# Block 0's convolution as five sets of turned products instead of seven, with a new order of the first loads

## The reference

```python
w = exp(weight_gen - max); w = w / (sum(w) + 1e-09)      # over the 7 taps
out[b, s, h, :] = sum_k w[b, s, h, k] * x_pad[b, s + k, h, :]   # 6 rows of zeros in front
```

## Time and profile before

| what | us |
|---|---|
| median of 3 runs | 1212.82 |
| the profiled execution, its own time | 1212.99 |
| its span, first to last instruction | 1211.2 |
| TensorE (PE) busy in the span | 1194.2 |
| VectorE (DVE) busy | 880.5 |
| ScalarE (ACT) busy | 631.2 |
| GpSimd (POOL) busy | 41.7 |

### The profile page before, as it was taken

One profiled execution on the slowest core, in us unless ns is written; L12 is line 12 of the kernel. 1 busy time (PEld: TensorE's weight loads), 2 busy tenths in 40 slices (PEclk: granted clock), 3 DMA queues, 4 the chain that ended last, 5 costly groups with the idle time before them and its releaser, 6 DMA issues.

```text
span 1211.2 us, 26409 instructions
## 1 busy us (share of the span) xinstructions
PE 1194.2 (99%) x10524; PEld 1067.7 (88%) x10524; DVE 880.5 (73%) x1334; ACT 631.2 (52%) x1096; POOL 41.7 (3%) x38
## 2 busy tenths in 40 slices
PE   8999999999999999999999999999999999999998
PEld 7768789999988998999899988888989899998876
DVE  5887796776868778686776868778686776865565
ACT  4455645546364554645546364554645546364555
POOL 4431000000000000000000000000000000000000
PEclk9999999999999999999999999999999999999999
DMA  6332002020110202002020110202002020100000
GB/s 180 103 99 64 1 10 69 1 77 1 27 51 4 74 1 62 17 10 68 1 77 1 17 61 4 75 1 60 18 10 68 1 77 2 22 24 4 11 10 18
DMA packets 77636, 44.87 MB, mean 37 GB/s; under 512 B 54246, under 2 KB 69862, under 8 KB 77412
## 3 DMA queue, kind: packets, MB, share of 16 engines
q1 hardware_dynamic: 77396, 43.29, 13.4%
q10 hardware_dynamic: 144, 0.11, 0.0%
HBM read 31.58 MB, written 11.80 MB: 36 GB/s over the span
## 4 chain that ended last, share of the span: by engine, by line
PE 92%; DVE 5%; ACT 2%; issue 1%; DMA 0%; ACTq 0%
PE up_bank L891 34%; PE acc L906 23%; PE up_bank L897 17%; PE acc L913 16%; DVE hid_lo L739 1%; PE acc L1242 1%; DVE hidden L734 1%; DVE prod_even L624 1%; DVE hidden L731 1%; DVE sum_even L628 0%; ACT hidden L494 0%; DMA taps<-in_weight_gen_dram 0%; DVE prod_odd L624 0%; DVE taps L301 0%; DVE tap_max L610 0%
## 5 line engine op out<-in xcount | busy, mean ns | idle before, releaser
L891 PE MATMUL up_bank<-in_hi,up_hi 64*128 64x512 f32 x1280 | 356.6, 392 | 9.3 <-DVE hidden L731 5.3
L891 PE MATMUL up_bank<-in_lo,up_hi 64*128 64x512 f32 x1280 | 353.1, 387 | 0.0
L891 PE MATMUL up_bank<-in_hi,up_lo 64*128 64x512 f32 x1280 | 353.0, 387 | 0.0
L906 PE MATMUL acc<-hid_hi,dn_hi 64*128 64x512 f32 x872 | 337.3, 387 | 0.3 <-DVE hid_lo L739 0.2
L913 PE MATMUL acc<-hid_hi,dn_tail 64*128 64x512 f32 x872 | 337.3, 387 | 0.1
L906 PE MATMUL acc<-hid_lo,dn_hi 64*128 64x512 f32 x872 | 336.8, 386 | 0.0
L913 PE MATMUL acc<-hid_lo,dn_tail 64*128 64x512 f32 x872 | 336.8, 386 | 0.0
L906 PE MATMUL acc<-hid_hi,dn_lo 64*128 64x512 f32 x872 | 336.8, 386 | 0.0
L734 DVE SCALAR_TENSOR_TENSOR hidden<-hidden,up_bank 128x512 f32<-128x512 f32 x256 | 176.1, 688 | 199.7 <-ACT hidden L494 199.7
L739 DVE TENSOR_TENSOR hid_lo<-hidden,hid_hi 128x512 fp32r<-128x512 f32 x448 | 310.9, 694 | 1.0
L494 ACT ACTIVATE hidden<-up_bank,half_col 128x512 f32<-128x512 f32 x256 | 176.4, 689 | 226.4 <-DVE hid_lo L739 163.4
(11 more groups left out here) (117 smaller groups left out, 1398.8 us busy)
## 6 DMA issues: line engine op xcount, KB each, us to landing
window<-in_x_dram SPq DMA_DIRECT2D x14, 960.0 KB
out_dram<-out_rows SPq DMA_DIRECT2D x360, 16.0 KB, 1.5
turned_dram<-in_turned SPq DMA_DIRECT2D x56, 96.0 KB, 4.6
out_main<-turned_dram SPq DMA_DIRECT2D x14, 256.0 KB, 2.8
in_tail<-turned_dram SPq DMA_DIRECT2D x28, 128.0 KB, 3.0
stage<-in_moe_w_out_dram SPq DMA_DIRECT2D x7, 384.0 KB, 3.5
taps<-in_weight_gen_dram SPq DMA_DIRECT2D x1, 1456.0 KB, 8.5
stage<-in_moe_w_in_dram SPq DMA_DIRECT2D x4, 256.0 KB, 4.4
```

What stands on the lines that cost most here:

```text
L891: return nc.tensor.matmul(dst[:, :], w[lane[half], col:col + P], a[lane[half], :], start=first and product == 0, stop=False)
L906: return nc.tensor.matmul(acc[y][0], w[lane[half], k, :], a[lane[half], n % RING, :], start=half == LOW and product == 0 and k == 0, stop= ...
```

## The change

- The seven products reach TensorE as five sets: taps 6, 5 and 4 alone, then the sums of 3 and 2 and of 1 and 0. Of a pair the first product goes to PSUM (`z`, in the banks `up_bank2` and `up_bank3`, now one tile `up_pair1`), the second to SBUF, and VectorE adds them in SBUF. The normalised taps lie behind `z`, half of them in each of the two banks.
- Product order is now from the last tap to the first. The halo comes in two parts of 3 rows, near and far, each by one DMA a batch; tap 5 waits for the near part, the pair (3, 2) for the far one.
- The taps of block 0 are issued by SP ahead of the window instead of by ScalarE.
- No warm-up slot between the sets; `WARM_SLOTS` is 10 instead of 16.
- ScalarE casts weight pieces 0 to 4 before it reads the banks (before: 0 to 2, then the exponentials for blocks 1 and 2 and the Silu table, then 3 and 4), then piece 5, these exponentials, the table, and piece 6.
- `shift_early` follows the whole of block 0's convolution on VectorE.
- SP's load of block 1's window waits for the fifth set.

```diff
-WARM_SLOTS = 16
+WARM_SLOTS = 10
...
-        up_bank = [ctx.enter_context(nc.psum_tensor(f"up_bank{u}", [P, COLS], F32)) for u in range(4)]
+        up_pair = [ctx.enter_context(nc.psum_tensor(f"up_pair{u}", [P, 2, COLS], F32)) for u in range(2)]
+        up_bank = [up_pair[u // 2][:, u % 2, :] for u in range(4)]
...
-        first_taps = up_bank[3][:, 0:TAPS]
+        SUMS, TAPS2 = STEPS * D // 2, TAPS // 2
+
+        def sums_in(pair):
+            return pair[:, :, 0:SUMS].rearrange("p a (h g) -> p a h g", g=G)
+
+        def taps_in_banks(pair):
+            return pair[:, :, SUMS:SUMS + TAPS2].rearrange("p a (h k) -> p a h k", k=K)
+
+        def by_step_pair(ap):
+            return ap.rearrange("p (a h g) -> p a h g", a=2, g=G)
+
+        first_sets = [(6,), (5,), (4,), (3, 2), (1, 0)]
...
             def load_window0():
 
+                sp.dma_start(taps[:, 0:TAPS], taps_by_p[:, 0:TAPS]).then_inc(s_taps0, 16)
                 sp.dma_start(window[:, HALO * D:], x_by_p[:, 0:STEPS * D]).then_inc(s_window0, 16)
-                for e in range(B):
-                    p0, row0 = e * BATCH_P, e * S
-                    rows = x_rows[row0 + TPP - HALO:row0 + TPP - HALO + (BATCH_P - 1) * TPP, :]
-                    sp.dma_start(window[p0 + 1:p0 + BATCH_P, 0:HALO * D],
-                                 rows.rearrange("(p t) d -> p (t d)", t=TPP)[:, 0:HALO * D]).then_inc(s_halo0, 16)
+                for first, landed_halo in ((HALO // 2, s_halo_near), (0, s_halo_far)):
+                    for e in range(B):
+                        p0, row0 = e * BATCH_P, e * S + TPP - HALO + first
+                        rows = x_rows[row0:row0 + (BATCH_P - 1) * TPP, :].rearrange("(p t) d -> p (t d)", t=TPP)
+                        sp.dma_start(window[p0 + 1:p0 + BATCH_P, first * D:(first + HALO // 2) * D],
+                                     rows[:, 0:HALO // 2 * D]).then_inc(landed_halo, 16)
...
-            sp.wait_ge(s_product0, K)
+            sp.wait_ge(s_set0, len(first_sets))
...
-            act.dma_start(taps[:, 0:TAPS], taps_by_p[:, 0:TAPS]).then_inc(s_taps0, 16)
             act.wait_ge(s_half, 1)
             nc.scalar.activation(warm[:, 0:1], half_col[:, :], ACT.Exp)
             act.wait_ge(s_shifted, 1)
             exponentials(0, TAPS)
-            for q in range(3):
+            for q in range(OWN - 2):
                 weight_hi(q)
+            input1_hi_banks(0)
+            weight_hi(OWN - 2)
             act.wait_ge(s_shifted, 2)
             exponentials(TAPS, EARLY * TAPS)
             nc.scalar.activation(warm[:, 1:2], half_col[:, :], ACT.Silu)
-            for q in range(3, OWN - 2):
-                weight_hi(q)
-            input1_hi_banks(0)
-            for q in range(OWN - 2, OWN):
-                weight_hi(q)
+            weight_hi(OWN - 1)
             periods(act, period)
...
+                z, zt = sums_in(up_pair[1]), taps_in_banks(up_pair[1])
...
-                product(w_psum, K - 1, first_products[0]).then_inc(s_product0, 1)
-                dve.wait_ge(s_halo0, B * 16)
-                dve.wait_ge(s_halo_zero, 2)
-                for k in range(1, K):
-                    if k == K - 1:
-                        shift_early()
+
+                def product0(j, dst):
+                    return nc.vector.tensor_tensor(dst, by_step_pair(window[:, j * D:(j + STEPS) * D]),
+                                                   zt[:, :, :, j:j + 1].to_broadcast([P, 2, HEADS // 2, G]), ALU.mult)
+
+                for k, members in enumerate(first_sets):
+                    rows = by_step_pair(first_products[k % len(first_products)][:, :])
+                    if k == 0:
+                        dve.wait_ge(s_window0, 16)
+                    if members[0] == HALO - 1:
+                        dve.wait_ge(s_halo_near, B * 16)
+                        dve.wait_ge(s_halo_zero, 2)
+                    if members[-1] == HALO // 2 - 1:
+                        dve.wait_ge(s_halo_far, B * 16)
                     wait(dve, s_turned0, k - len(first_products) + 1)
-                    product(w_psum, k - 1, first_products[k % len(first_products)]).then_inc(s_product0, 1)
+                    if len(members) == 1:
+                        product0(members[0], rows).then_inc(s_set0, 1)
+                    else:
+                        dve.wait_ge(s_set0, k)
+                        product0(members[0], z).then_inc(s_part0, 1)
+                        product0(members[1], rows).then_inc(s_part0, 1)
+                        dve.wait_ge(s_part0, 2 * (k - 2))
+                        nc.vector.tensor_tensor(rows, z, rows, ALU.add).then_inc(s_set0, 1)
...
             conv_block0()
+            shift_early()
             input1_lo_banks(0)
...
-                for k in range(K):
-                    pe.wait_ge(s_product0, k + 1)
+                for k in range(len(first_sets)):
+                    pe.wait_ge(s_set0, k + 1)
                     rows = first_products[k % len(first_products)][:, :].rearrange("p (t d) -> p t d", t=STEPS)
                     add_turned(k, rows, slice(0, P), main_banks(0))
                     mm = add_turned(k, rows, slice(P, D), tail_banks)
-                    if k < K - 1:
+                    if k < len(first_sets) - 1:
                         mm.then_inc(s_turned0, 1)
-                        keep_warm(1)
```

More of the change, by code:

```diff
@@ L183, in swiglu_hardswish_kernel @@
         s_window0 = sem("s_window0")
-        s_halo0 = sem("s_halo0")
+        s_halo_near = sem("s_halo_near")
+        s_halo_far = sem("s_halo_far")
         s_taps_rest = sem("s_taps_rest")
@@ L215, in swiglu_hardswish_kernel @@
         s_norm0 = sem("s_norm0")
-        s_product0 = sem("s_product0")
+        s_part0 = sem("s_part0")
+        s_set0 = sem("s_set0")
         s_turned0 = sem("s_turned0")
@@ L656, in conv_block0 @@
                 dve.wait_ge(s_norm0, 3)
-                w_psum = first_taps.rearrange("p (c k) -> p c k", k=K)
-                nc.vector.tensor_tensor(w_psum, w, denom[:, :].unsqueeze(2).to_broadcast([P, HEADS, K]),
-                                        ALU.mult).then_inc(s_norm0, 1)
+                z, zt = sums_in(up_pair[1]), taps_in_banks(up_pair[1])
+                nc.vector.tensor_tensor(zt, w.rearrange("p (a h) k -> p a h k", a=2),
+                                        denom[:, :].rearrange("p (a h) -> p a h", a=2).unsqueeze(3).to_broadcast(
+                                            [P, 2, HEADS // 2, K]), ALU.mult).then_inc(s_norm0, 1)
@@ L660, in conv_block0 @@
                 dve.wait_ge(s_norm0, 4)
-                dve.wait_ge(s_window0, 16)
-                product(w_psum, K - 1, first_products[0]).then_inc(s_product0, 1)
-                dve.wait_ge(s_halo0, B * 16)
-                dve.wait_ge(s_halo_zero, 2)
-                for k in range(1, K):
-                    if k == K - 1:
-                        shift_early()
-                    wait(dve, s_turned0, k - len(first_products) + 1)
-                    product(w_psum, k - 1, first_products[k % len(first_products)]).then_inc(s_product0, 1)
+                def product0(j, dst):
+                    return nc.vector.tensor_tensor(dst, by_step_pair(window[:, j * D:(j + STEPS) * D]),
+                                                   zt[:, :, :, j:j + 1].to_broadcast([P, 2, HEADS // 2, G]), ALU.mult)
@@ L1243, in add_turned @@
                                               ident[lane[half], lane[half]], start=k == 0 and t == 0,
-                                              stop=k == K - 1 and t == STEPS - 1)
+                                              stop=k == len(first_sets) - 1 and t == STEPS - 1)
                 return mm
             def turn_products0():
-                for k in range(K):
-                    pe.wait_ge(s_product0, k + 1)
+                for k in range(len(first_sets)):
+                    pe.wait_ge(s_set0, k + 1)
                     rows = first_products[k % len(first_products)][:, :].rearrange("p (t d) -> p t d", t=STEPS)
```

## The result

| | before | changed |
|---|---|---|
| median, us | 1212.82 (8 runs) | 1207.44 (8 runs) |
| lowest to highest | 1212.50 to 1213.08 | 1207.12 to 1210.69 |
| profiled execution, its own time | 1212.99 | 1208.50 |
| its span | 1211.2 | 1206.4 |
| mean granted clock of that span | 1.000 | 0.998 |

The ratio is 0.9961, with a 95% interval of 0.9950 to 0.9972: 0.4% faster, as forecast in sign and nearly in size (1208.0). What was not forecast is the spread. Five runs lie between 1207.12 and 1207.58 at a clock of 0.999 or 1.000, and three at 1208.50, 1209.61 and 1210.69 with 0.998, 0.997 and 0.997.

A forecast was written before the change was run, and what follows sets the result against it. The prediction took TensorE to set the pace at the start, up to the banks' reading at 21.83 us. It summed 1212.99 - 5.15 + 0.36 = 1208.2, less 0.17: 1208.0 us, range 1206.7 to 1210.4.

The forecast's parts named there:

- Step 1: Start, block 0's taps: they land at 3.6 us instead of 5.06, so the first product starts at 6.35.
- Step 2: Halo in two parts: near half needs no wait at 7.2 us; far half is awaited until 9.3.
- Step 3: VectorE's products and adds: adds take 0.95 us each, bounded by 1.90; the pairs are ready at 12.1 and 14.9.
- Step 4: TensorE's sets: banks full at 16.65 us instead of 21.80, 5.15 gained, 1.3 idle before the fifth set.
- Step 5: ScalarE's list behind the banks: first Silu waits for ScalarE, 0.36 us late; GpSimd's later weights stay hidden.
- Step 6: After the start: the shift is kept through 62 us and beyond; one VectorE-GpSimd meeting more or less is 0.95 us.
- Rivals A and B: A: first DMAs no faster, 1209.1 us, chance 0.15; B: gain partly given back at 15 to 62 us, 1209.9, 0.13.
- Rival C: TensorE's clock stays low or falls in the gaps: 11 us lost against 4.8 gained, 1219 us, chance 0.04.

The follow-up runs named there:

- e9: e5 with 18 warm-up slots ahead of the first set and two after the fourth: 1209.24 us, ratio 0.9970.
- e6: Changed kernel with the halo in one part, waited for ahead of the second product: 1215.16 us, ratio 1.0016.
- e3: Changed kernel with ScalarE's casts of weights 5, 6 and 7 moved after the second Silu and the first rounding: 1210.22 us.
- e8: Changed kernel with the first product of each pair in an SBUF tile instead of PSUM: 1210.02 us, ratio 0.9977.
- e12: The changed kernel itself, measured again: 1208.51 us, ratio 0.9965.
- e2: Changed kernel with 16 warm-up slots instead of 10: 1208.12 us, ratio 0.9962.
- e7: Changed kernel with seven single sets without adds instead of five sets: 1209.62 us, ratio 0.9976.
- e11: Changed kernel with one warm-up slot after the first and fourth sets each, and ScalarE's casts of weights 5 to 7 moved again: 1208.86 us, ratio 0.9967.
- e1: Changed kernel with two warm-up slots after the fourth set: 1208.05 us, ratio 0.9964.
- e4: Changed kernel with the later casts of e3 and the filled gap of e1 together: 1209.56 us.
- e5: Changed kernel with block 0's taps issued by ScalarE's queue again: 1215.79 us, ratio 1.0018.
- e10: The kernel before the change with 10 warm-up slots instead of 16: 1224.18 us, ratio 1.0074.

## Why the prediction was right, and where its sizes were off

**Step 1** (taps at 3.6): right in kind, too late by 0.7 us. They land at 2.86 (0.73 + 2.13), at the lower bound of 2.8. The estimate by the Trainium skill's page "DMA: Bandwidth & Descriptors", 3.0, was the nearer one, though the page gives its table for DMAs that GpSimd issues. The text held that an earlier landing would change nothing, as the far halo would be awaited: that was the error, next step. e9 prices the landing at 1.4 to 2.0 us.

**Step 2** (near half in time, far half awaited at 9.3): the near half was in time, the far half too. Both products behind it started without a wait for a DMA at 6.48 and 8.40; taking 9.3 as the far half's landing, from the undivided halo's 9.11, was too cautious. In e6 the undivided halo itself is in by 8.00. Why it comes earlier is not shown: the taps have left the second queue, and the weights behind the halo are issued 1.2 us later (3.15 against 1.95). The margin is small, as the profile of e3 has a wait of 0.17 us for the far half.

**Step 3** (adds at 0.95): measured 0.96 in PSUM and 1.81 and 1.40 in SBUF (e8); the upper bound of 1.90 was the price of the form that the change avoids. Two starts were mis-sized, as each pair waits for the end of the set before it: the first pair starts 1.05 us after the product before it, not 0.87, and the second 1.06 after the add before it, not 0.96. That cost 0.3 us.

**Step 4** (5.15 us of the banks' time, 1.3 us idle): measured 5.89 and 0.89, the latter 0.28 in e12's profile. Sets are 1.65 us apart, not 1.45; the 1.45 between two warm-up slots had left the overlap of their ends in the slots' 0.42. As VectorE sets the pace, this cost nothing and made the gap smaller. That TensorE no longer sets the pace is shown by its wait before the fifth set, by that set's start at 14.18 in two runs whose first sets lie 0.3 us apart, and by e6, where a VectorE that is 1.5 us late gives banks that are 1.5 us late. It is close behind: in e2 and e7, with more of TensorE's work ahead of the banks, it sets the pace again.

**Step 5** (Silu 0.36 late): at full clock 5.01 us after the banks instead of 4.79, 0.22 late, with no wait for TensorE, and e3 and e11 bring it back to 4.80 and 4.77. The mechanism was right; the insert overlaps a little better. Weights 3 and 4 were cast by 14.6, ahead of the banks. The claim that the later GpSimd work is hidden held, but by a small margin, as e3 and e11 showed. In the profiled run the first Silu starts at 21.87 where the prediction had 21.8, and block 1's first product 4.76 us earlier than before where it had 4.8 (32.36 against 37.12). Both agree by luck: the banks came 0.7 us earlier than forecast, and the low clock took 0.9 back, with a wait of Silu for TensorE that the prediction had ruled out. At full clock, in e12, they start at 20.96 and 31.48.

**Step 6** (the shift lasts): VectorE's list from 28 to 57 us has the same meetings as before, and the table above the same 27.67 us.

The sum with the measured terms is 1212.82 - 5.89 + 0.22 = 1207.15 us, and the lowest run took 1207.12. The forecast was 0.85 us above this: 0.7 for the banks (taps 0.7 and far half 0.3 too late, the two starts 0.3 too early) and 0.14 for Silu. The median, 1207.44, lies 0.56 below the forecast, as the spread took 0.3 back; in e12 it took more, and the median of 1208.51 lies above. So part of the nearness to 1208.0 is luck. Rivals A and B did not come: the loads were early, the adds took 0.96, and the meetings are the same.

**Rival C** was given 0.04 as an all-or-nothing loss of 11 us. The mechanism is real and is in the measurement: 6 of the 13 runs of the changed kernel are at 0.997 or 0.998 and pay 1 to 3.5 us of span. What was wrong was the argument against it, that TensorE ran at full rate after 0.75 us of idle time in the kernel before and that dense sets then keep the clock up. There the 0.75 us stand alone ahead of 13 us of work; here 0.89 us stand ahead of one set, and 0.69 follow. Counting a clock of 0.998 or less as a fall, kernels with a gap before the fifth set and no filler (the change twice, e3) fell in 14 of 24 runs, kernels with that gap filled or closed (e1, e2, e4, e7, e9, e11) in 2 of 43. In e8, with gaps of 0.97 and 1.38 us, all ten runs fell. These counts go by the records of the clock, which e5 and e10 show to be incomplete. That idle time of TensorE in this stretch causes it is shown by this, e3 against e4 above all, and by e5 against e9. Why a given run is spared is not shown. The gap's length alone does not decide it: of the profiled runs with ten slots and no filler, those of e12, e3 and e6 were spared with 0.28, 0.48 and 1.20 us before the fifth set, and the changed kernel's first one fell with 0.89. The Trainium skill's "TensorE: Matmul & The Clock Gate" (Part 1) says that the throttled state is the default and sustained activity releases it. The first half agrees with e10, where 1.92 us of idle time are followed by 27 us at 0.5; the second does not, as TensorE was busy for 20.98 of 21.00 us there and stayed at 0.53. The measurement decides.

**Open.** Runs at full clock still differ, by 1.2 us in e1 (1207.29 and 1208.50), 1.5 in e2 (1207.17 and 1208.62) and 1.0 in e7, whose TensorE has no idle time there. A fall that the records miss is one possible reason. The profile of e4 shows another: the second product waited 0.90 us for the near halo. With TensorE no longer in front of it the start now depends on when DMAs land; that this explains the other runs was not shown. The filler is shown to change the clock; in time it gives 0.7 us between the medians of e3 and e4, and none that was shown against the changed kernel. No version was shown to beat the change: e1 and e2 have ratios of 0.9964 and 0.9962, inside its interval, and only a lower top (1209.00 and 1208.62 against 1210.69, in five runs against eight). The dropped slots between the sets were not run by themselves; their 1.3 us are the estimate under e7.

## What to carry to other kernels

Where TensorE sums products at the pace of another engine, let that engine do just enough of the adding that both finish together, and keep the other operand in PSUM while GpSimd is at work. Put the small load that heads the chain first in the queue, and split a load where its first user needs only half. Then look at the idle time that the new order gives TensorE: run it with the gaps filled by matmuls that nobody reads, and look at the clock of every run, not only the profiled one. Here the clock fell with gaps of 0.9 to 2 us, and a fall cost 1 to 11 us, up to more than the whole rearrangement brought.

## What the runs showed that was not expected

- After 2 us without work TensorE ran at half clock for 20.5 us (e5) and 27 us (e10) although it was busy nearly all that time; the price was 6.5 and 11 us.
- The DMA of 112 KB at the head of SP's queue landed in 2.1 us; from ScalarE's queue beside a load of 384 KB it took 4.3 (before) and 4.1 (e5).
- The same 40 warm-up records ended between 6.53 (e5) and 7.14 us (e12), 0.6 us apart with nothing changed in them.
- The time between the span and the time of a run is 1.8 us in most runs, and up to 2.9 (e12's profiled run: 1208.32 with a span of 1205.4).
